# Order of ScalarE's and VectorE's work in the first MLP stage: bank copies ahead of weights' casts, three sums sooner

## Chip, core and metric

One core of a Trainium2 chip runs the whole program. The metric is the device time of one execution in microseconds. Of the kernel before there are three timed runs and one profiled execution.

## What is computed

Three layers in a row, all in float32: an attention with decaying state, an MLP with squared relu, and an MLP with a gate behind an RMS norm. The change touches the first MLP. Cut to what matters:

```python
# attention: B, H, S, D = 4, 8, 768, 64; its output is x, 3072 tokens x 512
h = np.maximum(x @ w_in, 0.0)           # w_in 512 x 2048
x = h * h @ w_out                       # w_out 2048 x 512
# second MLP: rms norm, silu(xn @ w_gate) * (xn @ w_val) @ w_out, 3072 x 512, d_ff 1536
```

## The kernel before

**Products.** Each MLP works on three tiles of 1024 tokens. A front run multiplies a tile by a block of the first weights, a back run multiplies the hidden values by the second weights. A run splits its matrices into two by two blocks and needs only seven products of blocks (a Strassen-like scheme, in the form of Winograd): some operands are sums of blocks, and results are shared between products by adding further products into the same bank. The first MLP has four front runs for each tile and then one back run. The runs in question are the first four front runs, numbered 0 to 3 (also m = 0 to 3), and the back run behind them.

**High and low parts.** Every float32 operand is split in two: ScalarE casts it to the fast matmul format (the high part, `high_w`, `high_front`, `high_quad`, `high_hop`), and another engine subtracts the cast from the operand (the low part). For the weights of a front run GpSimd does it (`low_w`, L706), for tokens and items VectorE. A product of blocks is then twelve matmuls, three for each of four pairs of blocks (L862 to L864). Product k of the next run's weights goes to the place in `w_ops` that product k of this run has read, so a cast of `high_w(m + 1, k)` waits for product k of run m (L976).

**Banks.** Products 0 to 6 go to X, Z, Y, X, Y, Z, Y. Between them the banks are copied:
- ScalarE copies X to Y after product 0 (`seed`, L1045); product 2 waits for it, and it waits for VectorE's last multiply of the run before (L1596).
- ScalarE copies Z to `p5` after product 1 (`save_p5`, L1058).
- ScalarE copies Y to `u2` after product 2 (`save_u2`, L1065); product 4 waits for it.
- After product 3 ScalarE takes the relu of X (L1164) and VectorE multiplies it by X (L1627).
- After product 4 VectorE adds Y and p5 into `hid` block Dd (L1631, `c22_done`); product 6 waits for it. ScalarE then takes relu and square of that block (L1196, L1198).
- After product 5 VectorE adds Z and u2 (L1641) and squares its relu (L1582).
- After product 6, at the head of the next run, ScalarE takes the relu of Y (`tail`, L1092) and VectorE multiplies (L1596).

**Sums of weights.** Four of the seven weight operands are sums of blocks (`sum_w`, L1479, L1481, L1484, L1487 on VectorE). `sum_w(m, i)` makes the operand of product 1, 4, 2 or 5 for i = 0, 1, 2, 3.

**Items of the second weights.** The seven operands of each of seven groups ("quads") of second weights are made once, split into high and low part, and stored in DRAM as items, to be loaded in each back run. Quads 0 and 1 are made in the attention; quads 2 and 3 in runs 1 to 3. Their work is cut into eleven units, dealt out over the slots of a run by `units_at`: VectorE does sums (L1500, L1502, L1506, L1510) and low parts (L1516), ScalarE the casts (`high_quad`, L1017), SyncE the stores (L465). Run 2 has in slot 2 the last two items of quad 2 and the first sum of quad 3, in slot 3 the second sum and the first item of quad 3. Run 1 has in slot 2 a sum and two items, in slot 3 a sum and one item. Run 3 has in slot 2 two items and a sum, in slot 3 two items. SyncE loads the items of the back run (L512) only behind the last store of its queue.

**Order.** Each engine works its own queue strictly in the order in which the code issues it, written out by hand in `front_run` for ScalarE (L1112) and `front1_run` for VectorE (L1613). `prep(slot)` deals out casts of weights and tokens, `quads(slot)` item casts. In run 0 the token operands of products 3 to 6 are still to be cast (`high_front`), the last two after stores out of the same places have landed; run 0 works at the casts of run 1's weights, runs 1 to 3 at those of the next run.

ScalarE's order in runs 1 to 3 before:

```python
save_p5(run)
quads(1)
prep(2)         # high_w(m + 1, 1)
save_u2(run)
quads(2)
prep(3)         # high_w(m + 1, 2)
```

Of the kernel before, what the change touches and what calls it, by code (L numbers as in the profile page):

```python
# [33 lines left out]
R1, R2 = Q1 // 2, Q2  # L34
# [102 lines left out]
def build(nc, qkv, decay_rows, tables, w_f1, w_f2, w_b, rms_g, out):  # L137
# [6 lines left out]
    with ExitStack() as ctx:  # L144
# [799 lines left out]
        def _(act):  # L944
# [137 lines left out]
            def tail(run):  # L1082

                if run < RUNS1:
                    t, i = divmod(run, R1 + 1)
                    if i < R1:
                        if t:
                            act.wait_ge(y_stored[i], 16 * t)
                        if t == 0 and i == R1 - 1:
                            act.wait_ge(kept3[3], 16)  # L1090
                        act.wait_ge(*done(run, 6))
                        nc.scalar.activation(hid[:, 2 * i:2 * i + 2, C, :], Y[:], ACT.Relu).then_inc(relu_y, 1)  # L1092
                    else:
                        act.wait_ge(*done(run, 6))
                        act.wait_ge(squares_added, 5 * t + 4)
                        nc.scalar.activation(gt[:], Y[:], ACT.Square).then_inc(squared, 1)
                        scale_y(Y, C, y_taken)
                    return
                t, i = divmod(run - RUNS1, R2 + 1)
                if i < R2:  # L1100
                    silu(run, 3)
                elif t == TILES - 1:
                    for i, tb in enumerate(LAST_BLOCKS):
                        act.wait_ge(last_done, i + 1)
                        nc.scalar.activation(by_column(out_sb[:, C, tb, :]), in_rows(tokens(Y)[:, tb, :]), ACT.Copy,
                                             scale=rinv_t[:, tb:tb + 1]).then_inc(last_scaled, 1)
                else:
                    act.wait_ge(*done(run, 6))
                    nc.scalar.copy(out_sb[:, C].rearrange("p t d -> p (t d)"),
                                   Y[:].rearrange("p z n -> p (z n)")).then_inc(y_taken, 1)  # L1110

            def front_run(run, m, fresh, front, bk=None):  # L1112

                more = m + 1 < MS
                t, second = front_tile(front)

                def prep(slot):
                    if more and slot and m:
                        high_w(m + 1, slot - 1)
                    if fresh and slot < 4:  # L1120
                        high_front(front, 3 + slot)

                def quads(slot):
                    for quad, unit in units_at(m, slot + 1) if slot < 6 else units_at(m + 1, 0):
                        if unit_item(unit) is not None:
                            high_quad(quad, unit_item(unit))

                if run:
                    tail(run - 1)
                if m:  # L1130
                    high_w(m, 6)
                if m == 1:
                    for i in range(3):
                        act.wait_ge(x_stored[i], 16 * len(stored_chunks()[i::3]))
                if run == 0:
                    seed(run)
                    prep(0)
                else:
                    prep(0)
                    seed(run)  # L1140
                quads(0)
                prep(1)
                save_p5(run)
                quads(1)
                prep(2)
                save_u2(run)
                quads(2)
                prep(3)
                if m == 0:
                    high_w(1, 0)  # L1150
                    high_w(1, 1)
                quads(3)
                if not second:
                    i = m % R1
                    if i == R1 - 1:
                        for j in range(4):
                            act.wait_ge(kept[j], 16 * len(range(j, 7 * (1 + t), 4)))
                    if m == 1:
                        act.wait_ge(early_kept[EARLY_PLACES - 1], 16)
                    if m == 2:  # L1160
                        for j in (0, 1, 2, 3, EARLY_PLACES - 2):
                            act.wait_ge(early_kept[j], 16)
                    act.wait_ge(*done(run, 3))
                    nc.scalar.activation(hid[:, 2 * i:2 * i + 2, A, :], X[:], ACT.Relu).then_inc(relu_x, 1)  # L1164
                elif not fresh:
                    silu(run, 0)
                if m == 0:
                    high_w(1, 2)
                    high_w(1, 3)
                prep(4)  # L1170
                quads(4)
                if second and fresh:
                    silu(run, 0)
                    silu(run, 1)
                if m == 0:
                    high_w(1, 4)
                prep(5)
                quads(5)
                if bk:
                    high_hop(bk, 0)  # L1180
                if second and not fresh:
                    silu(run, 1)
                if m == 0:
                    high_w(1, 5)
                prep(6)
                if bk:
                    high_hop(bk, 1)
                    if second:
                        high_hop(bk, 2)
                if second:  # L1190
                    silu(run, 2)
                quads(6)
                if not second:
                    h = hid[:, 2 * i:2 * i + 2, Dd, :]
                    act.wait_ge(c22_done, run + 1)
                    nc.scalar.activation(h, h, ACT.Relu).then_inc(relu_d, 1)  # L1196
                    act.wait_ge(relu_d, m + 1)
                    nc.scalar.activation(h, h, ACT.Square).then_inc(h_d, 1)  # L1198

            def root(t):  # L1200

# [94 lines left out]
            for t in range(TILES):  # L1296
                bk = BackRun(t, False)
                for p in range(R1):
                    front_run(run_f1(t, p), R1 * t + p, p == 0, t, bk if p == R1 - 1 else None)
                back_run(bk)  # L1300
            for t in range(TILES):
                bk = BackRun(t, True)
# [6 lines left out]
        def _(dve):  # L1309
# [209 lines left out]
            def prep(m, slot, fresh, front):  # L1519

                if 0 < m < MS - 1 and slot < 2:
                    sum_w(m + 1, 2 * slot)
                    if not fresh:
                        sum_w(m + 1, 2 * slot + 1)
                if fresh and slot < 4:
                    low_front(front, 3 + slot)
                    if slot == 0 and front == 0:
                        combine(front, 3)
                if m == 0 and slot in (1, 2):
                    sum_w(1, 2 * slot - 2)  # L1530
                for quad, unit in units_at(m, slot):
                    quad_unit(quad, unit)

# [79 lines left out]
            def front1_run(run, m, t, p, bk):  # L1613

                fresh = p == 0
                if run:
                    tail(run - 1)
                for slot in range(4):
                    prep(m, slot, fresh, t)
                if t and p == R1 - 1:  # L1620
                    fold(t - 1)
                if p == R1 - 1:
                    for j in range(4):
                        dve.wait_ge(kept[j], 16 * len(range(j, 7 * (1 + t), 4)))
                h = hid[:, 2 * p:2 * p + 2, A, :]
                dve.wait_ge(relu_x, m + 1)
                nc.vector.tensor_tensor(h, h, X[:], ALU.mult).then_inc(x_taken, 1)  # L1627
                prep(m, 4, fresh, t)
                dve.wait_ge(*done(run, 4))
                dve.wait_ge(p5_saved, run + 1)  # L1630
                nc.vector.tensor_tensor(hid[:, 2 * p:2 * p + 2, Dd, :], Y[:], p5[:], ALU.add).then_inc(c22_done, 1)  # L1631
                if fresh:
                    sum_w(m + 1, 1)
                    sum_w(m + 1, 3)
                if bk:
                    low_hop(bk, 0)
                dve.wait_ge(*done(run, 5))
                dve.wait_ge(u2_saved, run + 1)
                if m == R1 - 1:
                    dve.wait_ge(kept3[4], 16)  # L1640
                nc.vector.tensor_tensor(hid[:, 2 * p:2 * p + 2, Bb, :], Z[:], u2[:], ALU.add).then_inc(z_taken, 1)  # L1641
                relu_square(p, Bb, z_taken, run + 1, h_b)
                prep(m, 5, fresh, t)
                if bk:
                    low_hop(bk, 1)
# [252 lines left out]
```

## Time and profile before

| | |
|---|---|
| median of 3 runs | 1065.9 us (1065.86 to 1066.55) |
| profiled execution, its own time | 1065.99 us |
| its span, first to last instruction | 1064.2 us |
| TensorE clock granted, mean | 1.000 |
| TensorE busy | 1056.0 us, 5974 matmuls |
| VectorE busy | 877.6 us |
| ScalarE busy | 610.3 us |
| GpSimd busy | 332.7 us |
| chain of work that ended last | PE 93%, DMA 3%, POOL, DVE and ACT 1% each |

Busy times are sums over all instructions of an engine; a matmul's record overlaps that of the next, so the busy share of TensorE says that it is always occupied, not that it is at its peak. In the rows below, PE is TensorE, PEld its weight loads, DVE VectorE, ACT ScalarE, POOL GpSimd and SPq SyncE's queue of transfers. L numbers are lines of the kernel. A row of the timeline has start, duration, engine, line, operation, what is written and read, shapes, and a count; in brackets the idle time ahead of it and what ended it.

### The profile page before, as it was taken

What the parts mean: (1) busy time and instruction counts of PE and PEld (TensorE: products, weight loads), DVE (VectorE), ACT (ScalarE), POOL (GpSimd) and SP (SyncE); (2) the same over time, 40 slices, a digit from 0 to 9 for tenths busy, and PEclk for the clock granted to TensorE, in tenths of its full rate; (3) what the DMA queues carried; (4) which work ended last, traced back from release to release, by engine and by line L of the source; (5) the groups of instructions that cost most, each with busy time, mean ns of one, the idle gap of its engine ahead of it and who ended that gap; (6) DMA issues with size and microseconds to landing.
All of it is one profiled execution on the core that took longest, in us unless ns stands there. A gap on an engine that the chain in (4) does not pass through costs nothing.

```text
span 1064.2 us, 15678 instructions
## 1 busy us (share of the span) xinstructions
PE 1056.0 (99%) x5974; PEld 884.6 (83%) x5974; DVE 877.6 (82%) x940; ACT 610.3 (57%) x887; POOL 332.7 (31%) x244
## 2 busy tenths in 40 slices
PE   8999999999999999999999999999999999999998
PEld 7887788888888888888888888888888888888898
DVE  5896989878779878789899988978886986978684
ACT  4765775557664666654674645656454555544353
POOL 1864550004540015430034554005444102544000
PEclk9999999999999999999999999999999999999999
DMA  9999568664438644365642335632225751130455
GB/s 357 402 412 418 216 228 268 216 198 139 178 121 275 216 141 160 139 257 196 222 142 95 119 119 221 214 119 80 60 78 151 266 191 47 55 103 21 142 187 186
DMA packets 80553, 195.69 MB, mean 184 GB/s; under 512 B 24280, under 2 KB 34520, under 8 KB 75616
## 3 DMA queue, kind: packets, MB, share of 16 engines
q1 hardware_dynamic: 78016, 189.96, 51.4%
q10 hardware_dynamic: 2464, 4.74, 1.2%
q8 instruction: 48, 0.79, 0.3%
q14 instruction: 25, 0.20, 0.1%
HBM read 152.11 MB, written 42.48 MB: 183 GB/s over the span
## 4 chain that ended last, share of the span: by engine, by line
PE 93%; DMA 3%; POOL 1%; DVE 1%; ACT 1%; issue 0%; SPq 0%; ACTq 0%; POOLq 0%; DVEq 0%
PE Y L862 13%; PE Y L864 13%; PE Y L863 13%; PE Z L864 8%; PE Z L862 8%; PE Z L863 8%; PE X L864 8%; PE X L863 8%; PE X L862 8%; DMA item_scratch<-ops 2%; DMA raw_w<-w_b 1%; PE Z L813 1%; POOL ops L748 1%; PE X L785 1%; PE Y L785 1%; PE R L836 1%
## 5 line engine op out<-in xcount | busy, mean ns | idle before, releaser
L706 POOL TENSOR_TENSOR w_ops<-raw_w,w_ops 128x512 fp32r<-128x512 f32 x90 | 128.6, 1429 | 500.5 <-ACT w_ops L976 500.4
L1038 ACT CAST ops<-hid 128x1024 fp32r<-128x1024 f32 x147 | 154.7, 1053 | 162.8 <-PE Z L864 55.1
L1433 DVE TENSOR_TENSOR ops<-hid,ops 128x1024 fp32r<-128x1024 f32 x147 | 180.2, 1227 | 45.3 <-ACT ops L1038 44.8
L706 POOL TENSOR_TENSOR w_ops<-sums_w,w_ops 128x512 fp32r<-128x512 f32 x120 | 166.8, 1393 | 118.2 <-ACT w_ops L976 117.7
L862 PE MATMUL Y<-ops,w_ops 128*128 128x512 f32 x360 | 140.6, 391 | 0.5 <-ACT Y L1045 0.4
L864 PE MATMUL Y<-ops,w_ops 128*128 128x512 f32 x360 | 140.1, 389 | 0.0
L863 PE MATMUL Y<-ops,w_ops 128*128 128x512 f32 x360 | 140.1, 389 | 0.0
L1074 ACT ACTIVATE gt<-gt 128x512 f32<-128x512 f32 x72 | 45.1, 633 | 111.6 <-DVE gt L1650 38.9
L862 PE MATMUL Y<-ops 128*128 128x512 f32 (+1 forms) x288 | 104.5, 363 | 0.0
L863 PE MATMUL Y<-ops 128*128 128x512 f32 (+1 forms) x288 | 104.4, 362 | 0.0
L864 PE MATMUL Y<-ops 128*128 128x512 f32 (+1 forms) x288 | 104.4, 362 | 0.0
L976 ACT CAST w_ops<-sums_w 128x512 fp32r<-128x512 f32 x120 | 74.3, 621 | 42.6 <-PE Y L864 16.7
L862 PE MATMUL X<-ops,w_ops 128*128 128x512 f32 x240 | 93.5, 389 | 0.0
L864 PE MATMUL Z<-ops,w_ops 128*128 128x512 f32 x240 | 93.4, 389 | 0.0
L863 PE MATMUL X<-ops,w_ops 128*128 128x512 f32 x240 | 93.4, 389 | 0.0
L862 PE MATMUL Z<-ops,w_ops 128*128 128x512 f32 x240 | 93.4, 389 | 0.0
L863 PE MATMUL Z<-ops,w_ops 128*128 128x512 f32 x240 | 93.4, 389 | 0.0
L864 PE MATMUL X<-ops,w_ops 128*128 128x512 f32 x240 | 93.4, 389 | 0.0
L862 PEld LDWEIGHTS Y<-ops,w_ops 128*128 128x128 f32 x360 | 67.6, 188 | 16.3 <-ACT Y L1045 0.8
L1348 DVE TENSOR_TENSOR ops<-raw,ops 128x1024 fp32r<-128x1024 f32 x39 | 55.3, 1423 | 29.3 <-ACT ops L995 29.3
L864 PEld LDWEIGHTS Y<-ops,w_ops 128*128 128x128 f32 x360 | 67.6, 188 | 14.2
L863 PEld LDWEIGHTS Y<-ops,w_ops 128*128 128x128 f32 x360 | 67.6, 188 | 13.7
(180 smaller groups left out, 2320.3 us busy)
## 6 DMA issues: line engine op xcount, KB each, us to landing
ops<-item_scratch SPq DMA_DIRECT2D x147, 512.0 KB, 3.7
raw_w<-w_f SPq DMA_DIRECT2D x30, 1024.0 KB, 5.0
item_scratch<-hid SPq DMA_DIRECT2D x30, 512.0 KB, 3.1
qk_sb<-qkv SPq DMA_DIRECT2D x23, 512.0 KB, 8.6
kv_sb<-qkv SPq DMA_DIRECT2D x20, 512.0 KB, 9.5
y_scratch<-hid SPq DMA_DIRECT2D x12, 512.0 KB, 5.6
raw<-y_scratch SPq DMA_DIRECT2D x3, 2048.0 KB, 9.6
raw<-w_b SPq DMA_DIRECT2D x5, 1024.0 KB, 4.9
```

The costliest lines, as they stand in the source:

```text
L706: nc.gpsimd.tensor_tensor(w_ops[:, k, 1], front_w_source(m, k), f32(w_ops[:, k, 0]), ALU.subtract).then_inc(w_lo, 1)
L748: nc.gpsimd.tensor_tensor(place[:, 1], quad_source(quad, ITEMS[i]), f32(place[:, 0]), ALU.subtract)\
L785: mm = nc.tensor.matmul(scores_ps[n % 2][:, h % 2, cols], qk_sb[rows, n % QKR, KT, cols], qk_sb[rows, n % QKR, QT, cols], start=h < 2, sto ...
L813: mm = nc.tensor.matmul(y_place(n, h), kv_sb[:, n % KVR, V, h * D:(h + 1) * D], masked[:, c % 2, h % 2, P * p:P * p + P], start=c == 0 and ...
L862: nc.tensor.matmul(dst, left_hi, right_hi, start=start, stop=False, skip_group_check=True)
L863: nc.tensor.matmul(dst, left_hi, right_lo, start=False, stop=False, skip_group_check=True)
L864: return nc.tensor.matmul(dst, left_lo, right_hi, start=False, stop=True, skip_group_check=True)
L976: nc.scalar.copy(w_ops[:, k, 0], front_w_source(m, k)).then_inc(w_hi, 1)
L1038: nc.scalar.copy(hop_at(n)[:, 0], hid[:, 2 * g:2 * g + 2, OPERAND[k], :]).then_inc(hop_hi, 1)
L1074: nc.scalar.activation(gt[:, i % 2, :], gt[:, i % 2, :], ACT.Silu).then_inc(gate_out, 1)
L1348: nc.vector.tensor_tensor(front_lo_at(k), raw_slot(OPERAND[k]), f32(front_hi_at(k)), ALU.subtract).then_inc(front_lo, 1)
L1433: nc.vector.tensor_tensor(hop[:, 1], hid[:, 2 * g:2 * g + 2, OPERAND[k], :], f32(hop[:, 0]), ALU.subtract).then_inc(hop_lo, 1)
```

## The change

It does three things, all for the first MLP.

ScalarE in run 0 gets an order of its own (`first_run`): the copy into u2 directly behind that into p5, one weights' cast, then the two last token casts, then the relu of X, then four weights' casts, then relu and square of block Dd, then the last weights' cast. Before, the copy into u2 stood behind a token cast, two weights' casts stood ahead of the relu of X, and all six ahead of relu and square of Dd.

ScalarE in runs 1 to 3 (`m < R1`) copies into u2 directly behind p5, ahead of `quads(1)` and `prep(2)`. From run 4 on the order is as it was, with u2 behind `prep(2)`.

VectorE in run 0 makes three sums of run 1's weights in slot 1, ahead of the low parts of the token operands 5 and 6. Before, one stood in slot 1, one in slot 2, and one behind the add for product 6.

```diff
+            def raise_d(run, m):
+                h = hid[:, 2 * (m % R1):2 * (m % R1) + 2, Dd, :]
+                act.wait_ge(c22_done, run + 1)
+                nc.scalar.activation(h, h, ACT.Relu).then_inc(relu_d, 1)
+                act.wait_ge(relu_d, m + 1)
+                nc.scalar.activation(h, h, ACT.Square).then_inc(h_d, 1)
+
+            def first_run():
+                seed(0)
+                high_front(0, 3)
+                high_front(0, 4)
+                save_p5(0)
+                save_u2(0)
+                high_w(1, 0)
+                high_front(0, 5)
+                high_front(0, 6)
+                act.wait_ge(*done(0, 3))
+                nc.scalar.activation(hid[:, 0:2, A, :], X[:], ACT.Relu).then_inc(relu_x, 1)
+                for k in range(1, 5):
+                    high_w(1, k)
+                raise_d(0, 0)
+                high_w(1, 5)
...
                 quads(0)
                 prep(1)
                 save_p5(run)
+                if m < R1:
+                    save_u2(run)
                 quads(1)
                 prep(2)
-                save_u2(run)
+                if m >= R1:
+                    save_u2(run)
                 quads(2)
                 prep(3)
-                if m == 0:
-                    high_w(1, 0)
-                    high_w(1, 1)
                 quads(3)
...
@@ VectorE, prep
-                if m == 0 and slot in (1, 2):
-                    sum_w(1, 2 * slot - 2)
+                if m == 0 and slot == 1:
+                    sum_w(1, 0)
+                    sum_w(1, 2)
+                    sum_w(1, 1)
@@ VectorE, front1_run
                 if fresh:
-                    sum_w(m + 1, 1)
+                    if m:
+                        sum_w(m + 1, 1)
                     sum_w(m + 1, 3)
```

The rest of the diff takes the cases for run 0 out of ScalarE's `front_run` and calls `first_run` in its place.

## Rows read from the trace of the kernel before

**Rows 1.** The page, busy time of each engine (span share, instructions).

```profile
PE 1056.0 (99%) x5974; PEld 884.6 (83%) x5974; DVE 877.6 (82%) x940; ACT 610.3 (57%) x887; POOL 332.7 (31%) x244
```

**Rows 2.** Timeline of TensorE: first matmuls of runs 0 to 3 and the back run.

```profile
84.90 0.50 PE L862 MATMUL X<-ops,w_ops 128*128 128x512 f32 x1
...
104.77 0.39 PE L862 MATMUL X<-ops,w_ops 128*128 128x512 f32 x1
...
124.75 0.39 PE L862 MATMUL X<-ops,w_ops 128*128 128x512 f32 x1
...
143.79 0.39 PE L862 MATMUL X<-ops,w_ops 128*128 128x512 f32 x1
...
162.83 0.39 PE L862 MATMUL X<-ops 128*128 128x512 f32 x1
```

**Rows 3.** Waits from 84 to 165 us (us in total, times, longest).

```profile
PEld Y L862 <- ACT Y L1045: 0.8, 1, 0.8
...
PEld Y L862 <- ACT u L1065: 0.7, 2, 0.4
...
PEld Y L862 <- DVE hid L1631: 0.5, 1, 0.5
```

**Rows 4.** Timeline of TensorE: the two matmuls behind a wait in run 1.

```profile
110.77 0.50 PE L862 MATMUL Y<-ops,w_ops 128*128 128x512 f32 x1 [0.40 <-ACT Y L1045]
111.11 0.39 PE L863 MATMUL Y<-ops,w_ops 128*128 128x512 f32 x1
```

**Rows 5.** Timeline of ScalarE and VectorE in run 0.

```profile
94.03 1.05 ACT L995 CAST ops<-raw 128x1024 fp32r<-128x1024 f32 x1 [1.20 <-DMA item_scratch<-ops]
...
96.44 1.05 ACT L995 CAST ops<-raw 128x1024 fp32r<-128x1024 f32 x1 [0.45 <-issue]
...
100.63 1.22 DVE L1631 TENSOR_TENSOR hid<-Y,p 128x1024 f32<-128x1024 f32 x1
...
108.39 1.22 DVE L1596 TENSOR_TENSOR hid<-hid,Y 128x1024 f32<-128x1024 f32 x1 [0.22 <-ACT hid L1092]
```

**Rows 6.** Timeline of ScalarE in run 2, up to the copy into u2.

```profile
131.30 0.62 ACT L1017 CAST hid<-raw 128x512 fp32r<-128x512 f32 x1
132.01 0.62 ACT L1017 CAST hid<-gt 128x512 fp32r<-128x512 f32 x1
132.54 0.61 ACT L976 CAST w_ops<-sums_w 128x512 fp32r<-128x512 f32 x1
133.11 1.02 ACT L1065 COPY u<-Y 128x1024 f32<-128x1024 f32 x1
```

**Rows 7.** Timeline of VectorE and GpSimd in run 2, up to the add.

```profile
132.66 0.69 DVE L1516 TENSOR_TENSOR hid<-gt,hid 128x512 fp32r<-128x512 f32 x1
...
133.23 1.29 POOL L706 TENSOR_TENSOR w_ops<-sums_w,w_ops 128x512 fp32r<-128x512 f32 x1 [2.46 <-ACT w_ops L976]
133.39 1.68 DVE L1500 TENSOR_TENSOR gt<-raw 128x512 f32<-128x512 f32 x1
...
134.99 0.68 DVE L1502 TENSOR_TENSOR gt<-raw 128x512 f32<-128x512 f32 x1
135.24 1.58 POOL L706 TENSOR_TENSOR w_ops<-sums_w,w_ops 128x512 fp32r<-128x512 f32 x1 [0.72 <-ACT w_ops L976]
135.59 1.78 DVE L1516 TENSOR_TENSOR raw<-raw 128x512 fp32r<-128x512 f32 x1
...
137.29 1.21 DVE L1627 TENSOR_TENSOR hid<-hid,X 128x1024 f32<-128x1024 f32 x1
...
138.55 1.23 DVE L1631 TENSOR_TENSOR hid<-Y,p 128x1024 f32<-128x1024 f32 x1
```

**Rows 8.** Timeline of SyncE's queue, last store and the back run's first load.

```profile
155.76 0.33 SPq L465 DMA_DIRECT2D item_scratch<-raw  x1
156.71 0.32 SPq L512 DMA_DIRECT2D ops<-item_scratch  x1
```

**Rows 9.** Transfers issued from 156.6 to 156.9 us (size, us to landing).

```profile
ops<-item_scratch SPq DMA_DIRECT2D x1, 512.0 KB, 4.8
```

More of the change, by code:

```diff
@@ L1117, in prep @@
                 def prep(slot):
-                    if more and slot and m:
+                    if more and slot:
                         high_w(m + 1, slot - 1)
@@ L1126, in quads @@
                             high_quad(quad, unit_item(unit))
[L1128 to L1131, printed above, removed]
+                tail(run - 1)
+                high_w(m, 6)
                 if m == 1:
@@ L1134, in front_run @@
                         act.wait_ge(x_stored[i], 16 * len(stored_chunks()[i::3]))
[L1135 to L1140, printed above, removed]
+                prep(0)
+                seed(run)
                 quads(0)
@@ L1166, in front_run @@
                     silu(run, 0)
-                if m == 0:
-                    high_w(1, 2)
-                    high_w(1, 3)
                 prep(4)
@@ L1174, in front_run @@
                     silu(run, 1)
-                if m == 0:
-                    high_w(1, 4)
                 prep(5)
@@ L1182, in front_run @@
                     silu(run, 1)
-                if m == 0:
-                    high_w(1, 5)
                 prep(6)
@@ L1193, in front_run @@
                 if not second:
[L1194 to L1198, printed above, removed]
+                    raise_d(run, m)
             def root(t):
@@ L1298, in _ @@
                 for p in range(R1):
-                    front_run(run_f1(t, p), R1 * t + p, p == 0, t, bk if p == R1 - 1 else None)
+                    if t or p:
+                        front_run(run_f1(t, p), R1 * t + p, p == 0, t, bk if p == R1 - 1 else None)
+                    else:
+                        first_run()
                 back_run(bk)
```

## The prediction, made before the changed kernel was run

> **What bounds the kernel now.** I read the page first: TensorE is busy 99% of the span [rows 1]. So time can only come from places where its matmuls stop, and the next view is the timeline of TensorE. A front run is seven products of twelve matmuls. The first matmuls of the runs [rows 2] give run lengths of 19.87, 19.98, 19.04 and 19.04 us. The last two have no gap, so a clean product is 19.04 / 7 = 2.72 us. Runs 0 and 1 carry 0.83 and 0.94 us too much; 0.11 of it is the start at 84.90. Nothing like it comes later: I looked through all matmuls to the end and found no other gap. The waits [rows 3] name who is late: the seed copy (ACT Y L1045), the copy into u2 (L1065, twice) and VectorE's add of p5 (L1631). After such a wait the second matmul comes 0.34 us behind the first where 0.23 is usual, so a stop costs its lateness and 0.11 more [rows 4]; the rest of the excess suggests 0.15, which I use. **All that the change can take away is 1.77 - 0.11 = 1.66 us, 0.16% of the time.** I take 1.6.
>
> **What it takes away.** (1) Run 0, copy into u2. It sat behind a cast that waited for a store until 94.03 [rows 5]. It now starts when product 2 is done: 84.90 + 0.11 + 3 x 2.72 + 0.2 = 93.4, and ends at 94.4 (1.02 us [rows 6]). Product 4 is due at 95.9. (2) The add for product 6. ScalarE's relu of X no longer has two weights' casts (0.62 each) ahead of it; the last front cast (1.05) still waits for its store, until 96.44, so the relu starts at 97.4, VectorE's multiply at 98.7 and the add at 99.8, not 100.63 [rows 5]. It ends at 101.0; product 6 is due at 101.35. (3) Relu and square of Dd no longer wait behind the cast of sum 5, so the relu of Y starts when product 6 is done, 104.4. VectorE's multiply then waits only for its own square, which a hold by GpSimd draws out to 105.7, and starts there, not at 108.39 [rows 5]; the seed ends near 108.1 and is due at 109.6. (4) Run 1's u2 copy starts when product 2 is done (112.5) and ends 1.5 us before product 4. All four stops go.
>
> What pays for (1) to (3): three sums of 0.68 on VectorE ahead of the low parts of operands 5 and 6. The low part of 5 then ends by 97.6 (a hold of 0.45 by GpSimd included, see below) and is due at 98.6; that of 6 ends at 98.75, due at 101.35. If that cover of 1.0 us went, product 5 would be late by the difference. GpSimd's first low part comes 3 us earlier and SP's next weights' load with it; both have most of a run in hand. I cost these at nothing.
>
> **What it adds.** In runs 1 to 3 the u2 copy is moved ahead of two item casts and the cast of the next weights' operand 1. Look at run 2 [rows 6]: the casts ran at 131.30, 132.01 and 132.54, and the u2 copy started at 133.11, when product 2 was done (124.75 + 8.16 + 0.2 = 133.11). It was not late; the casts stood in time that ScalarE had free. Moved ahead of them, it blocks its queue until product 2 is done. Call the copy's start U: a copy takes 1.02 and the next instruction starts 0.09 before its end, so the first cast stands at U + 0.93, on the old clock 134.04, 2.7 us later than 131.30. Behind them VectorE works a chain that ends in the add for product 6: two items' low parts, two sums, one low part, multiply X, add [rows 7]. Before, the add started at 138.55 and ended at 139.78, with product 6 due at 143.79 - 2.72 = 141.07: 1.3 us of cover.
>
> Durations for the chain. A ScalarE cast is 0.62 and the next starts 0.53 behind it; a 512-wide VectorE instruction 0.68, the next 0.08 before its end; a GpSimd low part 1.29. But VectorE and GpSimd hold each other up [rows 7]: GpSimd ran 133.23 to 134.52, and VectorE's sum that began at 133.39 ended at 135.07, 0.55 behind it. GpSimd's 135.24 ended at 136.82, 1.15 behind VectorE's sum (135.67); the low part that began at 135.59 ended at 137.37, again 0.55 behind. Whoever asks second ends 0.55 (VectorE) or 1.15 (GpSimd) after the other, and they take turns. Instructions that read a bank, as 137.29 and 138.55, show no such thing.
>
> The Trainium skill (SBUF — State Buffer, section Who interferes with whom) has it that a Vector instruction with two SBUF inputs and a GpSimd instruction that reads SBUF contend, and calls the shared pair of ports an exclusive lock under which the other fully blocks. The rows agree on the blocking, but not on a full one: the blocked instruction ends less than its own duration after the other. By the rows the sum is the +2.9 below; by a full block it would be +4.5, which is rival D.
>
> Run 2, in us after U: item casts 0.93 and 1.46, weight cast 1.99 to 2.61. VectorE low parts 1.58 and 2.17 to 2.85. GpSimd asks at 2.65, ends 2.85 + 1.15 = 4.00. VectorE sum, asked at 2.9, ends 4.55. Next item cast 2.95 (it needs the second low part), weight cast 3.48 to 4.10; GpSimd asks at 4.18, ends 4.55 + 1.15 = 5.70. VectorE second sum ends 6.25. GpSimd's next (cast behind the relu of X, at 5.6) ends 7.40; VectorE's low part 7.95. Multiply 7.87, add 9.0 to 10.22, TensorE 10.27. Product 6 is due at U + 7.96. **Late by 2.30.** Run 1 has one sum, then one low part behind the two: 4.00, 4.55, 5.70, 6.25; multiply 6.17, add ends 8.52. **Late by 0.6.** Run 3: low parts to 2.85, GpSimd 4.00, sum 4.55; a cast of that sum 4.61, weight cast 5.14, relu of X 5.66 to 6.68, multiply 6.71, add ends 9.06. **Late by 1.15.** With 0.15 for each restart: 4.05 + 0.45 = 4.5.
>
> The multiplies, squares and low parts behind these adds shift with TensorE. One queue more: SP stores the last item once VectorE's last low part is done (155.76), and issues the back stage's first load behind it (156.71), which took 4.8 us [rows 8, 9], to 161.5, with product 0 of the back run at 162.83 [rows 2]. By the run 3 chain the last low part ends at U + 5.94, so the load is issued at U + 6.9 and lands at U + 11.7; TensorE gets there at U + 9.11 + 0.15 + 2.72 = 12.0. Hidden, by 0.3: nothing in the sum.
>
> **Sum:** -1.6 + 4.5 = +2.9 us. The profiled execution took 1065.99 us with a span of 1064.2; the median is 1065.9. Forecast 1065.9 + 2.9 = **1068.8**. For this kernel about 0.2%, 2.1 us, can be told from no change.
>
> **Rivals.** A, the forecast, 0.58. B, the other side: **the casts stay covered.** Without holds between VectorE and GpSimd the chains end at U + 7.0, 7.3 and 7.9, all before 7.96, and only the gain is left: 1064.3. It decides at 0.7 us of hold in run 2. For it: the three instructions meet at other moments than before, and a hold needs an overlap. Against it, [rows 7] show three holds in a row in the same part of VectorE's queue. 0.12. C, **one turn less in run 2**: GpSimd asks for its second turn 0.37 before VectorE's sum ends; asks it later, VectorE's second sum runs unheld, saving 1.1: 1067.7, and with such luck in run 1 too 1067.1. 0.18. D, **full blocks**: 0.13 to 0.14 more at each turn, four in run 1, six in run 2, two in run 3: +1.6, 1070.4. The rows speak against it. 0.05. E, **the first back-stage load lands late**: its cover is 0.3; were it 1 us slower than its 4.8, 0.7 and a restart come on top: 1069.6. 0.07. That the four stops don't go (the add in run 0 has only 0.3 of cover) would put 0.5 to 1.6 on top of any case; I leave it to the upper end.
>
> **The numbers.** Likeliest is A. The range leaves out B and the last of D: from C with two saved turns and a little, 1066.8, to D, 1070.2. Slower by over 0.2% is from 1068.03: most of A, D and E: 0.69. Within 0.2%: B, C and the low edge of A: 0.29. Faster needs under 1063.8, more than all the stops together: 0.02.
>
> **What would show it.** In the new profile, run 0 and run 1 should be without waits of TensorE on L1045 and the u2 copy; run 1's first product near 104.2. In runs 1 to 3 there should be one stop each, before product 6, on VectorE's add, of about 0.6, 2.3 and 1.15 us; the item casts should stand right behind the u2 copy. Wrong if runs 1 to 3 are 19.04 long (then B), or if the stop of run 2 is near 1.2 (C), or if the first product of the back run waits for a load (E).

## The result and the profile after

| | before | changed |
|---|---|---|
| median | 1065.86 us (6 runs, 1065.55 to 1066.55) | 1070.64 us (6 runs, 1070.10 to 1072.04) |
| ratio | | 1.0042, 95% interval 1.0031 to 1.0052 |
| profiled execution, its time and span | 1065.99, 1064.2 us | 1071.06, 1069.3 us |
| mean TensorE clock, all runs | 1.000 in the profiled one | 1.000 in four, 0.998 in two |

The change made the kernel 4.8 us slower (0.42%), where 2.9 had been forecast: the direction was right, the size was not, and the time lies 0.4 us above the range.

The page shows no difference by engine: TensorE still counts as busy in 99% of the span.

```profile
PE 1056.1 (99%) x5974; PEld 885.2 (83%) x5974; DVE 879.1 (82%) x940; ACT 609.9 (57%) x887; POOL 334.7 (31%) x244
```

The timeline of TensorE, changed kernel, first matmuls of runs 0 to 3 and of the back run, to be laid beside [rows 2]:

```profile
85.92 0.50 PE L862 MATMUL X<-ops,w_ops 128*128 128x512 f32 x1
...
105.09 0.39 PE L862 MATMUL X<-ops,w_ops 128*128 128x512 f32 x1
...
124.91 0.39 PE L862 MATMUL X<-ops,w_ops 128*128 128x512 f32 x1
...
146.41 0.39 PE L862 MATMUL X<-ops,w_ops 128*128 128x512 f32 x1
...
167.78 0.47 PE L862 MATMUL X<-ops 128*128 128x512 f32 x1 [0.46 <-DMA ops<-item_scratch]
```

The run lengths are 19.17, 19.82, 21.50 and 21.37 us, where they were 19.87, 19.98, 19.04 and 19.04. Run 0 got shorter by 0.70, run 1 by 0.16, runs 2 and 3 got longer by 2.46 and 2.33: together 3.93. The first product itself started 1.02 later in this execution. That lies in the attention stage, whose instructions are the same; the experiments below show how it scatters.

The waits between 84 and 170 us, changed kernel (us in total, times, longest), against [rows 3]:

```profile
PEld Y L862 <- DVE hid L1644: 5.3, 3, 2.6
PE Y L862 <- DVE hid L1644: 4.0, 3, 2.2
...
PE X L862 <- DMA ops<-item_scratch: 0.5, 1, 0.5
```

The seed copy and the copy into u2 are gone from TensorE's rows (PE and PEld). Three waits for one line have come: L1644 is the add that frees product 6 (L1631 before). One wait for a transfer came with them, that of the back run's first load. How run 2 got there is in the timeline of ScalarE, VectorE and GpSimd, changed kernel, beside [rows 6, 7]:

```profile
133.27 1.01 ACT L1065 COPY u<-Y 128x1024 f32<-128x1024 f32 x1 [1.71 <-PE Y L864]
134.18 0.62 ACT L1017 CAST hid<-raw 128x512 fp32r<-128x512 f32 x1
...
134.83 0.69 DVE L1527 TENSOR_TENSOR hid<-raw,hid 128x512 fp32r<-128x512 f32 x1 [2.77 <-ACT hid L1017]
135.44 0.69 DVE L1527 TENSOR_TENSOR hid<-gt,hid 128x512 fp32r<-128x512 f32 x1
136.16 1.67 DVE L1511 TENSOR_TENSOR gt<-raw 128x512 f32<-128x512 f32 x1
137.75 1.78 DVE L1513 TENSOR_TENSOR gt<-raw 128x512 f32<-128x512 f32 x1
139.45 1.77 DVE L1527 TENSOR_TENSOR raw<-raw 128x512 fp32r<-128x512 f32 x1
141.15 1.21 DVE L1640 TENSOR_TENSOR hid<-hid,X 128x1024 f32<-128x1024 f32 x1
142.28 1.21 DVE L1644 TENSOR_TENSOR hid<-Y,p 128x1024 f32<-128x1024 f32 x1
...
135.92 3.06 POOL L706 TENSOR_TENSOR w_ops<-sums_w,w_ops 128x512 fp32r<-128x512 f32 x2 [5.01 <-ACT w_ops L976]
138.94 1.74 POOL L706 TENSOR_TENSOR w_ops<-raw_w,w_ops 128x512 fp32r<-128x512 f32 x1
...
143.55 0.50 PE L862 MATMUL Y<-ops,w_ops 128*128 128x512 f32 x1 [2.16 <-DVE hid L1644]
```

ScalarE now idles 1.71 us ahead of the u2 copy and VectorE 2.77 us ahead of its first low part. Then three of VectorE's 512-wide instructions in a row take 1.67 to 1.78 us instead of 0.69, each of them held behind a low part of GpSimd's. With U = 133.27, the start of the copy, the add ends at U + 10.22, the number of the forecast. GpSimd's second low part ends at 138.98, U + 5.71, where 5.70 was forecast, so rival C (one turn less) did not come.

### The profile page after: what moved, and what is told of

It reads as the page before. It is cut to its first block, busy times and chain, and to the rows that moved or that the text cites. A ratio compares the mean times of both kernels' runs of the same rounds, so it can differ in the third digit from the quotient of the medians.

```text
span 1069.3 us, 15678 instructions
## 1 busy us (share of the span) xinstructions
PE 1056.1 (99%) x5974; PEld 885.2 (83%) x5974; DVE 879.1 (82%) x940; ACT 609.9 (57%) x887; POOL 334.7 (31%) x244
## 4 chain that ended last, share of the span: by engine, by line
PE 94%; DVE 3%; issue 1%; DMA 1%; ACT 0%; SPq 0%; ACTq 0%; DVEq 0%
PE Y L862 13%; PE Y L864 13%; PE Y L863 13%; PE X L862 8%; PE Z L864 8%; PE X L863 8%; PE Z L863 8%; PE X L864 8%; PE Z L862 8%; PE Z L813 1%; PE R L836 1%; PE Z L804 1%; PE X L785 1%; PE Y L785 1%; DVE masked L1344 1%
```

## The experiments

Besides the medians, each kernel is read from its trace as **span less start**: from TensorE's first product to the end. For the kernel before that is 1064.2 - 84.90 = 979.3 us, for the changed one 1069.3 - 85.92 = 983.4. It leaves the scatter of the attention stage out. The lengths of runs 0 to 3 say where it comes from; 19.04 is a run without a stop, and about 19.2 is a run 0 without one.

**1. The move of the u2 copy in no run.**

```diff
                 save_p5(run)
-                if m < R1:
-                    save_u2(run)
                 quads(1)
                 prep(2)
-                if m >= R1:
-                    save_u2(run)
+                save_u2(run)
```

> The changed kernel with the copy into u2 of runs 1 to 3 back behind the item casts and the weights' cast; run 0 as changed. My theory (all of the loss is in that move): the four stops of before are gone and none is new, so 1.4 to 1.6 us faster than the kernel before, about 1064.3, first matmul of run 1 0.6 us and of run 2 1.4 us nearer to that of run 0 than before. Rival 1 (part of the loss comes from run 0's new order or from an attention stage that the change slowed, whose end was 1.0 us later in the profile): TensorE's first product starts near 85.9 again and the time is 1065.3 or more.

Measured: ratio 0.9989 (0.9979 to 0.9999), medians 1065.51 and 1066.25. No wait of TensorE for any engine from its first product into the back run; lengths 19.21, 19.04, 19.04, 19.04; span less start 977.7, which is 1.6 below the kernel before, the number of the forecast. The gain in the median is 0.7, where 1.4 to 1.6 was forecast. In this trace the first product started at 85.44, 0.54 later than in that of the kernel before; the rest of the difference is not placed. The median alone would suit rival 1, the span less start doesn't. So the whole loss is in the move, and the other two parts of the change are a gain.

**2. The move alone, on the kernel before.**

```diff
                 save_p5(run)
+                if 0 < m < R1:
+                    save_u2(run)
                 quads(1)
                 prep(2)
-                save_u2(run)
+                if m == 0 or m >= R1:
+                    save_u2(run)
```

> The kernel before with only the copy into u2 of runs 1 to 3 moved ahead. My theory: the stops of run 0 and the seed's in run 1 stay, the small one of run 1's u2 copy goes (0.35), and before product 6 of runs 1 to 3 stand stops of 0.6, 2.3 and 1.6 us, then one of 0.6 for the back run's first load, 5.5 us with the restarts: 5.2 us slower than before, 1071.0. Rival 1 (run 0's order shares in the loss): less than 4.2 us slower.

Measured: ratio 1.0049 (1.0035 to 1.0062), medians 1072.22 and 1066.25, 6.0 apart. Span less start 983.75, 4.45 above the kernel before. The first product started at 84.75, the earliest of all, in the kernel with the longest median. The stops ahead of product 6 are as in the changed kernel; the one for the back run's load did not occur, which is why 4.45 came and not 5.2. The median is further away than the trace, in the main for the reason under 7 (three of the six executions had the lower clock; a fourth took 1072.53 at the full one).

**3. GpSimd kept out of VectorE's way.**

```diff
                 for k in range(6):
+                    if k == 1 and 0 < m < R1:
+                        pool.wait_ge(relu_x, m + 1)
                     if m + 1 < MS:
                         low_w(m + 1, k)
```

> The changed kernel, but GpSimd's low parts of weights' operands 1 to 5 in runs 1 to 3 wait for the relu of X, so that none meets VectorE's item chain; ScalarE's and VectorE's order untouched. My theory (the late casts alone would be covered, it is the holds between VectorE and GpSimd that make the add late): stops of runs 1 and 2 before product 6 gone, that of run 3 at most 0.4 us, no wait for the back run's load; 1064.3 to 1064.8. Rival 2 (the late casts are enough by themselves, GpSimd has no part): as the changed kernel, stops of 0.6, 2.3 and 1.6 us, about 1070.6. VectorE's 512-wide sums and low parts in that stretch should all take 0.68 to 0.70 us by my theory.

Measured: ratio 1.0021 (1.0013 to 1.0030), median 1068.68. Neither theory's number, but the trace tells why. Run 2, timeline of VectorE:

```profile
134.65 0.69 DVE L1529 TENSOR_TENSOR hid<-gt,hid 128x512 fp32r<-128x512 f32 x1
135.37 0.69 DVE L1513 TENSOR_TENSOR gt<-raw 128x512 f32<-128x512 f32 x1
135.98 0.69 DVE L1515 TENSOR_TENSOR gt<-raw 128x512 f32<-128x512 f32 x1
136.59 0.69 DVE L1529 TENSOR_TENSOR raw<-raw 128x512 fp32r<-128x512 f32 x1
137.47 1.22 DVE L1642 TENSOR_TENSOR hid<-hid,X 128x1024 f32<-128x1024 f32 x1 [0.20 <-ACT hid L1185]
```

ScalarE's and VectorE's order is the changed kernel's and the casts come as late, but the same three instructions take 0.69, and the stops ahead of product 6 in runs 1 and 2 are gone. That part of my theory holds, and rival 2 falls for these two runs. In run 3 a stop of 0.66 stays, where at most 0.4 was expected: that much the late casts cost there without a hold. What I had not expected is that the work that GpSimd put off came back: it held VectorE's squares and low parts later (two of them, 128x1024, took 2.33 and 2.32 us), so that the seed of run 3 was late by 0.74, and stops of 0.23 and 0.99 stood before the back run's first product and before a later one (length of run 3 20.97). Span less start is 981.1, 3.4 above experiment 1. With a restart of 0.15 for each, the four stops make 3.2 of it. Putting one engine off moved the collision; it did not remove it.

**4. The back run's first two loads ahead of the last two item stores.**

```diff
@@ SyncE, front_run
                 for slot in range(7):
+                    if m == R1 - 1 and slot == 3:
+                        items_kept()
+                        load_items(bk, 0, 2)
                     for quad, unit in units_at(m, slot):
```

In the back stage the loads then begin at the third for the first tile.

> The changed kernel with the back run's first two loads issued ahead of the last two item stores in SyncE's queue. My theory (the stop before the back run's first product is that load's, queued behind the last store): that stop goes, 0.7 us less than the changed kernel, about 1069.9. Rival 3 (the wait only moves, to the low part of the back run's first operand or its third load): no gain.

Measured: ratio 1.0039 (1.0024 to 1.0054), median 1070.90, spread 1069.27 to 1072.53. The wait for the load is gone, and no other stands before the back run's first product; the median shows nothing, since the executions differ by more than that. Its two shortest, 1069.27 and 1069.59, lie under the shortest of the changed kernel, 1070.10. But experiments 2 and 5 show that the wait can be missing with the old queue, so its absence in one trace proves little. The load's own rows, changed kernel, say more (SyncE's queue; then size and us to landing), beside [rows 8, 9]:

```profile
159.96 1.44 SPq L465 DMA_DIRECT2D item_scratch<-raw  x2
162.03 2.02 SPq L512 DMA_DIRECT2D ops<-item_scratch  x4
...
ops<-item_scratch SPq DMA_DIRECT2D x1, 512.0 KB, 5.6
```

Issued at 162.03, landed at 167.6; the product was due at 166.93 + 0.23 = 167.16 and came at 167.78, 0.62 late. The same load took 4.8 us before, 4.4 in experiment 2 and again in experiment 9, and 4.5 in the kernel with the move in run 3 alone, and none of these three kernels waited. With 4.5 us it would have landed at 166.5 here as well. Over the twelve traces whose queue has this order it took 3.7 to 5.6 us; what makes the difference is open (the transfer engines were busy for a share of 1.00 from 162 to 168 here, and 0.98 in the six us behind 156.5 in the kernel before). So the load is hidden or not by its own scatter, and cost 0.62 us in the one trace where it wasn't.

**5. The move in one run at a time** (`if m == 1`, `2` or `3` in place of `if m < R1`, and `!=` in place of `>=`).

> The changed kernel with the copy into u2 ahead in run 1 alone. My theory (each run's move costs its own stop, and they add): one stop before product 6 of run 1, 0.6 us and a restart, 0.7 more than with the move in no run; span less the start of TensorE's first product 978.4. Rival 4 (the stops feed each other: run 2's is long because run 1 pushed the work): run 2 or 3 also stop here.

> The changed kernel with the copy into u2 ahead in run 2 alone. My theory: one stop before product 6 of run 2, 2.3 us, 2.4 more than with the move in no run; span less start 980.1 where the clock holds. Theory of the clock (a stop of over 2 us lets TensorE's clock fall for a few us in part of the executions, at 0.23 us more per matmul or some 2 us in all): some of the executions here have a mean clock of 0.998 and are some 1.5 to 2.5 us longer. Rival 4: the stop of run 2 is shorter by over 0.5 without that of run 1.

> The changed kernel with the copy into u2 ahead in run 3 alone. My theory: a stop before product 6 of run 3 of 1.6 us, and behind it 0.6 for the back run's first load, 2.3 with the restarts; span less start 980.0. By the theory of the clock, with no stop over 2 us, all or nearly all executions at a mean clock of 1.000. Rival 5 (the clock falls in any kernel as often, the stops have no part in it): 0.998 here and in the run 1 kernel as often as in the run 2 kernel.

| move in | median | ratio | lengths of runs 0 to 3 | span less start | at clock 0.998 |
|---|---|---|---|---|---|
| run 1 | 1065.84 | 0.9994 (0.9985 to 1.0003) | 19.19, 19.81, 19.04, 19.04 | 978.4 | 0 of 11 |
| run 2 | 1068.72 | 1.0023 (1.0014 to 1.0032) | 19.22, 19.04, 23.04, 19.12 | 981.7 | 6 of 11 |
| run 3 | 1066.83 | 1.0004 (0.9995 to 1.0013) | 19.17, 19.04, 19.04, 20.74 | 979.7 | 0 of 11 |

The before median of these rounds is 1066.52. Each move makes its own stop and no other: rival 4 falls, the gaps ahead of product 6 are 0.85, 2.54 and 1.80 us between two matmuls that otherwise stand 0.23 apart, and 0.85, 2.55 and 1.79 in the changed kernel with all three. The wait for the load did not come in the run 3 kernel. The run 2 kernel was profiled in an execution at a lower clock; without 1.6 us for that (7) it is 980.1.

**6. VectorE's three sums alone, on the kernel before.**

```diff
-                if m == 0 and slot in (1, 2):
-                    sum_w(1, 2 * slot - 2)
+                if m == 0 and slot == 1:
+                    sum_w(1, 0)
+                    sum_w(1, 2)
+                    sum_w(1, 1)
...
                 if fresh:
-                    sum_w(m + 1, 1)
+                    if m:
+                        sum_w(m + 1, 1)
                     sum_w(m + 1, 3)
```

> The kernel before with VectorE's three sums in run 0's slot 1 and nothing else. My theory: the weights' casts no longer wait for the sums, relu and square of Dd and so the relu of Y come earlier; the seed's stop in run 1 and that of its u2 copy go, the two stops of run 0 (u2 copy, add before product 6) stay: 1.0 us less than the kernel before, span less start 978.3. Rival (ScalarE's order alone brings the gain): all four stops stay, 979.3.

Measured: ratio 0.9990 (0.9981 to 0.9999), median 1065.36 beside 1066.52. Lengths 19.31, 19.04, 19.04, 19.04; span less start 977.8, where 978.3 was forecast. The seed's stop and that of run 1's u2 copy went, as expected. Of the two stops in run 0, which I had expected to stay, only 0.1 us is left of 0.7, with ScalarE's order as before. Here is why one of them vanished (ScalarE in run 0 of this kernel):

```profile
94.94 1.06 ACT L995 CAST ops<-raw 128x1024 fp32r<-128x1024 f32 x1 [1.17 <-DMA item_scratch<-ops]
95.90 1.00 ACT L1065 COPY u<-Y 128x1024 f32<-128x1024 f32 x1
```

The store landed 8.5 us after the first product (86.43), where it was 9.1 in [rows 5] (94.03 - 84.90). The u2 copy's lateness in run 0 hangs on how the attention stage ends, not on the order alone. So the sums alone bring nearly all of the gain. What ScalarE's new order in run 0 adds is 0.1 us here. It may be more where the stores land late; neither that nor ScalarE's order without the sums was tried.

**7. The clock.** Experiments 2 and 5 and the two rounds of the changed kernel answer what the medians hide. The run 2 kernel, TensorE behind its stop:

```profile
143.69 0.50 PE L862 MATMUL Y<-ops,w_ops 128*128 128x512 f32 x1 [2.15 <-DVE hid L1644]
...
144.50 0.40 PE L862 MATMUL Y<-ops,w_ops 128*128 128x512 f32 x1
144.73 0.60 PE L863 MATMUL Y<-ops,w_ops 128*128 128x512 f32 x1
145.12 0.63 PE L864 MATMUL Y<-ops,w_ops 128*128 128x512 f32 x1
145.54 0.63 PE L862 MATMUL Y<-ops,w_ops 128*128 128x512 f32 x1
```

and by windows (length; busy time of TensorE with its count; granted clock; share and GB/s of the transfers):

```profile
141.00:143.00 2.00, 0.54 (x3) 1.00 0.40 162
143.00:145.00 2.00, 1.31 (x5) 0.94 0.25 100
145.00:147.00 2.00, 2.00 (x6) 0.50 0.04 8
147.00:149.00 2.00, 2.00 (x8) 0.71 0.63 252
```

TensorE had been busy without a gap, stopped for 2.3 us, and ran again for 1.0 us; then its clock fell to half, 1.2 GHz, and the matmuls stood 0.43 apart instead of 0.23, eight of them: 8 x 0.20 = 1.6 us. The traces of experiments 4 and 9 show the same stretch behind the same stop, 1.6 and 1.1 us after the restart; the first trace of the changed kernel and that of experiment 2 have the stop and no such stretch. In this kernel the median of the executions at a full clock is 1068.02, of the others 1069.65, 1.6 more. Counted over all kernels with run 2's stop of 2.3 us (the changed one twice, experiments 2 and 4 and the run 2 kernel), 16 of 34 executions had the lower mean clock; over the other changed kernels 1 of 78, the stop of 1.57 us in the run 3 kernel among them (0 of 11); over the kernel before 2 of 77. Rival 5 falls.

**8. One cast put back: the weights' cast, or the item casts.**

```diff
@@ the weights' cast ahead of the u2 copy, the item casts behind it
                 save_p5(run)
                 if m < R1:
+                    prep(2)
                     save_u2(run)
                 quads(1)
-                prep(2)
                 if m >= R1:
+                    prep(2)
                     save_u2(run)
```

> The changed kernel, with only the cast of the next weights' operand 1 put back ahead of the copy into u2 in runs 1 to 3; the item casts stay behind it, as late as in the changed kernel. My theory (the first hold comes from GpSimd's low part of that cast meeting VectorE's item chain, and the later holds follow from the first): GpSimd does that part while ScalarE waits for product 2, the chain's first sum takes 0.69, no stop in runs 1 and 2, 0.1 to 0.6 in run 3, nothing for the load: span less start 977.8 to 978.5, and no execution at a lower clock. Rival 2 (the item casts' lateness is what costs): stops of 0.6, 2.3 and 1.6 us nearly as they are, 982.7 or more.

Measured: ratio 0.9999 (0.9990 to 1.0007), median 1066.44 beside 1066.51; span less start 978.8; lengths 19.18, 19.04, 19.04, 20.00; 0 of 11 at a lower clock. The span less start is 0.3 above the forecast's upper end, by the stop of run 3. The item casts stand right behind the u2 copy, as in the changed kernel. Run 2, ScalarE, VectorE and GpSimd:

```profile
131.07 0.62 ACT L976 CAST w_ops<-sums_w 128x512 fp32r<-128x512 f32 x1
132.88 1.01 ACT L1065 COPY u<-Y 128x1024 f32<-128x1024 f32 x1 [1.19 <-PE Y L864]
...
135.05 0.69 DVE L1528 TENSOR_TENSOR hid<-gt,hid 128x512 fp32r<-128x512 f32 x1
135.77 0.69 DVE L1512 TENSOR_TENSOR gt<-raw 128x512 f32<-128x512 f32 x1
136.38 0.68 DVE L1514 TENSOR_TENSOR gt<-raw 128x512 f32<-128x512 f32 x1
136.98 0.68 DVE L1528 TENSOR_TENSOR raw<-raw 128x512 fp32r<-128x512 f32 x1
...
131.77 1.29 POOL L706 TENSOR_TENSOR w_ops<-sums_w,w_ops 128x512 fp32r<-128x512 f32 x1 [1.23 <-ACT w_ops L976]
136.99 1.83 POOL L706 TENSOR_TENSOR w_ops<-sums_w,w_ops 128x512 fp32r<-128x512 f32 x1 [3.93 <-ACT w_ops L976]
```

GpSimd did its part at 131.77, while ScalarE waited for product 2 and VectorE for the casts behind it, and the chain ran without one hold. One cast of 0.62 us, placed nearly 4 us earlier against the copy, took the 2.3 us stop of run 2 away, and that of run 1. GpSimd's next low part still starts 4.1 us behind the copy (136.99), and by then the chain is at its last instruction: with the first hold the later ones went too. In run 1 the second hold stays (1.78 for the low part at 117.41), and one alone is covered. In run 3 a stop of 0.67 stays, as in experiment 3.

```diff
@@ the item casts ahead of the u2 copy, the weights' cast behind it
                 save_p5(run)
+                quads(1)
                 if m < R1:
                     save_u2(run)
-                quads(1)
                 prep(2)
```

> The changed kernel, with the item casts put back ahead of the copy into u2 in runs 1 to 3 and only the weights' cast left behind it. My theory: no stop in runs 1 to 3, as with the copy in its old place; span less start 977.7, no lower clock. Rival 6 (the weights' cast behind the copy is enough to bring the collision): stops before product 6 in runs 1 to 3 of 0.5 us or more.

Measured: ratio 0.9987 (0.9978 to 0.9996), median 1065.32 beside 1066.51: 1.2 us under the kernel before, and the lowest of all, though experiment 6 with 1065.36 is no worse. Lengths 19.17, 19.04, 19.04, 19.04, span less start 977.6, no wait of TensorE in runs 0 to 3. Rival 6 falls. From experiment 1 it can't be told apart (977.7). So in runs 1 and 2 neither the late item casts nor the late weights' cast stops TensorE by itself; it takes both behind the copy.

**9. The changed kernel again.**

> The changed kernel once more, for its spread. My theory: stops of 0.6, 2.3 and 1.6 us before product 6 of runs 1 to 3 as in its first profile, whatever the start of TensorE's first product (84.7 to 86.8 in the profiles so far, in no order of kernels); the stop for the back run's load in some executions and not in others, by how long that load takes (5.6 us in the first profile, 4.4 and 4.5 in two kernels with the same queue); mean clock 0.998 in a third to a half of the executions. Rival 1 (the change slows the attention stage): its first product starts at 85.9 or later again.

Measured: ratio 1.0041 (1.0029 to 1.0054), medians 1071.54 and 1066.51, 5 runs, three of them at 0.998. The profiled one is one of these: span less start 984.45, or 982.85 without 1.6 for the clock; no wait for the load. Its first product started at 85.35. Over the twelve traces other than that of the kernel before, starts lie between 84.75 and 86.80, the changed kernel's at 85.92 and 85.35, those of the kernels with medians below the one before at 85.44, 86.00, 86.20, 86.30 and 86.43. As rival 1 was put (85.9 or later again) it falls: the attention stage scatters by 2 us, whatever comes behind it. With one trace for most kernels, a shift of some tenths is not ruled out.

## Why the prediction fell short

**What it takes away: right.** All four stops went, 1.6 us (experiment 1: 979.3 to 977.7). The seed and u2 copies vanished from the waits. In run 0 of the changed kernel the u2 copy starts 8.5 us after the first product and the add for product 6 14.9 us after it, and the seed of run 1 ends 23.25 us after it; 8.5, 14.9 and 23.2 were forecast. That the two stops of run 0 would need ScalarE's order was not right in general: the sums alone did nearly the same (experiment 6).

**What it adds, runs 1 and 2: right, to a tenth.** Late by 0.6 and 2.30 was forecast. The gaps in the changed kernel are 0.85 and 2.55 between matmuls, less the usual 0.23: 0.62 and 2.32. The lengths give 0.78 and 2.46 with the restart, forecast 0.75 and 2.45. The turns between VectorE and GpSimd were taken as written, one after the other; experiments 3 and 8 show that they, and not the casts' lateness alone, carried these two stops.

**Run 3: a term too small.** "Late by 1.15" was 1.56. The step that failed is "a cast of that sum 4.61": I priced the hand-over from VectorE's sum to ScalarE's cast at 0.06 us. The sum itself ended where it was forecast, at U + 4.55 (U = 154.78 here). The hand-over took 0.37, in the changed kernel

```profile
154.78 1.01 ACT L1065 COPY u<-Y 128x1024 f32<-128x1024 f32 x1 [1.71 <-PE Y L864]
...
157.74 1.59 DVE L1521 TENSOR_TENSOR gt<-raw,gt 128x512 f32<-128x512 f32 x1
...
159.70 0.62 ACT L1017 CAST raw<-gt 128x512 fp32r<-128x512 f32 x1 [1.82 <-DVE gt L1521]
```

(159.33 to 159.70), 0.37 in experiment 8 where nothing is held, and 0.36 before the change, where I could have read it. Why this one hand-over is so slow is open. The relu's to the multiply took 0.13 where I had 0.03; that makes the 0.4. For the most part by the same two terms rival B's chain of run 3, "7.9", was wrong: unheld it ends 0.66 us late (experiments 3 and 8).

**The load: the step "Hidden, by 0.3: nothing in the sum" failed.** The margin was right and the price was not: I took one landing time, 4.8 us, as fixed. The issue and the due time moved together, and 4.8 us would still have been hidden, by 0.3 (162.03 + 4.8 = 166.83, due at 167.16). It was 5.6 in the changed kernel's first trace, and cost 0.62. With 4.4 in its second trace, and 4.4 and 4.5 in two other kernels, it cost nothing. Rival E, at 0.07, was the very case of the first trace. Of the twelve landing times (experiment 4), two are above the 5.1 us that were covered, so its chance was put too low.

**What no step had: the clock.** In 5 of 11 executions of the changed kernel the stop of 2.3 us brought a stretch at half clock, 1.6 us. The kernel before had no stop of such a length, and I did not ask what one does.

Added up, from the traces: run lengths +3.93 in place of +2.9 (0.4 for run 3, 0.62 for the load). By itself that would lie within the range, at 1069.8. The median of the six runs is 4.8 higher, 0.9 more than the run lengths; the clock in two of the six, and the attention stage's scatter of up to 2 us, can fill that, but how much each puts into the median is not settled. The range left the clock out and leaned on a single landing time; it was too narrow at its upper end.

The weighing of the lock was right. The Trainium skill (SBUF — State Buffer, section Who interferes with whom) says that whoever is second blocks fully. The traces disagree in the size: by full blocks run 2 would have been late by 3.1 (six turns of 0.13 to 0.14 on top of 2.30), by the rows 2.30, and it was 2.32.

## What to carry to other kernels

When a copy that must wait is moved ahead of work that need not, ask what stood in the waiting time: here ScalarE's casts did, and behind them two engines' work that had been spread out was pushed together. Two engines that hold each other turned one late start into a row of holds here, and moving one small instruction into the wait undid the stops of runs 1 and 2. A margin against a transfer is only as good as the spread of its landing time, and a stop is priced with what the clock does behind it.

## What was not expected of the hardware

- A stop of TensorE of 2.3 us, after about 19 us or more without a gap, was followed 1.0 to 1.6 us after the restart by some 3.4 us at 1.2 GHz in three of five traces. The lower mean clock that goes with it stood in 16 of 34 executions; behind a stop of 1.57 us it stood in none of 11. What lies between was not tried.
- The same load of 512 KB, in the same place of the same queue, landed in 3.7 to 5.6 us over twelve traces.
- Holding GpSimd back (experiment 3) moved its collisions with VectorE to another place. Of the 3.4 us above experiment 1, 2.7 are left without the 0.66 of run 3, and the three stops there, with their restarts, make 2.4 of them.
